# Attention's k-v product by head: two 65-column products on 64-column weight tiles in place of one 130-column product for a pair of heads

## What is computed

```python
q_s = exp(q - max(q, axis=-1)); q_s = q_s / (sum(q_s, axis=-1) + 1e-9)
k_s = exp(k - max(k, axis=2));  k_s = k_s / (sum(k_s, axis=2) + 1e-9)
kv  = np.einsum('bhsd,bhse->bhde', k_s, v)        # per head: 64x576 times 576x64
out = np.einsum('bhsd,bhde->bhse', q_s, kv)
# x = out as [4608, 512]
h = x @ w_in;  x = (h - tanh(h)) @ w_out           # [512, 2048], [2048, 512]
# then every row goes to the expert with the largest cosine, relu(x @ w1[e]) @ w2[e], times its gate
```

## Time and profile before

| | |
|---|---|
| median of 3 runs | 1547.14 us (1544.88 to 1548.52) |
| span of the profiled execution | 1546.1 us |
| TensorE matmul busy | 1464.8 us, 95% |
| TensorE weight load busy | 1275.8 us, 83% |
| VectorE busy | 979.8 us, 63% |
| ScalarE busy | 638.6 us, 41% |
| GpSimd busy | 406.7 us, 26% |

### The profile page before, as it was taken

One profiled execution on the slowest core, in us unless ns is written; L12 is line 12 of the kernel. 1 busy time (PEld: TensorE's weight loads), 2 busy tenths in 40 slices (PEclk: granted clock), 3 DMA queues, 4 the chain that ended last, 5 costly groups with the idle time before them and its releaser, 6 DMA issues.

```text
span 1546.1 us, 26526 instructions
## 1 busy us (share of the span) xinstructions
PE 1464.8 (95%) x7596; PEld 1275.8 (83%) x7597; DVE 979.8 (63%) x2003; ACT 638.6 (41%) x1268; POOL 406.7 (26%) x348
## 2 busy tenths in 40 slices
PE   4789999999999999999999999996999999999996
PEld 3678988989898988998898989985888888888885
DVE  8988677888778887867787876766422422432221
ACT  4454444455444454445444544443322322332220
POOL 3343233433323343323343332221000000001000
PEclk9799999999999999999999999997999999999999
DMA  8532011222001122101122000105421411411110
GB/s 194 145 93 78 1 45 31 57 49 54 16 15 48 33 64 47 45 2 45 31 55 51 23 14 14 62 15 183 148 78 43 142 48 41 146 41 41 47 39 25
DMA packets 139488, 90.85 MB, mean 59 GB/s; under 512 B 118872, under 2 KB 119128, under 8 KB 139232
## 3 DMA queue, kind: packets, MB, share of 16 engines
q1 hardware_dynamic: 132784, 70.12, 17.0%
q0 software_dynamic: 5840, 18.92, 3.2%
q10 hardware_dynamic: 736, 0.29, 0.1%
HBM read 70.39 MB, written 21.28 MB: 59 GB/s over the span
## 4 chain that ended last, share of the span: by engine, by line
PE 69%; DVE 19%; issue 6%; ACT 3%; POOL 0%; SPq 0%; DVEq 0%; DMA 0%; ACTq 0%; POOLq 0%
PE ps L510 20%; PE ps L511 20%; PE ps L512 20%; DVE gs L926 3%; DVE gs L923 2%; PE ps L683 2%; DVE big L921 2%; DVE gs L931 2%; PE ps L603 2%; PE ps L580 2%; DVE kfold L952 2%; DVE k_sb L960 1%; PE ps L597 1%; PE ps L662 1%; DVE qrec L945 1%
## 5 line engine op out<-in xcount | busy, mean ns | idle before, releaser
L1285 POOL TENSOR_TENSOR g_lo<-gs,g_hi 128x384 fp32r<-128x384 f32 x192 | 215.4, 1122 | 324.9 <-ACT g_hi L752 324.4
L510 PE MATMUL ps<-x_hi,wi_hi 128*128 128x384 f32 x768 | 279.8, 364 | 0.2 <-issue 0.2
L511 PE MATMUL ps<-x_lo,wi_hi 128*128 128x384 f32 x768 | 264.1, 344 | 0.0
L512 PE MATMUL ps<-x_hi,wi_lo 128*128 128x384 f32 x768 | 263.6, 343 | 0.0
L510 PE MATMUL ps<-wo_hi,g_hi 128*128 128x512 f32 x576 | 231.0, 401 | 13.4 <-POOL g_lo L1285 13.1
L511 PE MATMUL ps<-wo_lo,g_hi 128*128 128x512 f32 x576 | 229.4, 398 | 0.0
L512 PE MATMUL ps<-wo_hi,g_lo 128*128 128x512 f32 x576 | 227.8, 396 | 0.0
L752 ACT CAST g_hi<-gs 128x384 fp32r<-128x384 f32 x192 | 98.1, 511 | 287.2 <-DVE gs L931 285.3
L921 DVE TENSOR_SCALAR big<-usq 128x384 uint8<-128x384 f32 x192 | 117.0, 609 | 138.4 <-ACT usq L757 135.7
L861 ACT ACTIVATE hb<-ps 128x512 f32<-128x512 f32 x74 | 44.2, 597 | 314.6 <-PE ps L512 314.6
L1354 POOL DMA_INDIRECT out<-osb,xrow x37 | 36.2, 980 | 438.4 <-DVE osb L1258 429.5
(11 more groups left out here) (200 smaller groups left out, 2738.5 us busy)
## 6 DMA issues: line engine op xcount, KB each, us to landing
w_raw<-w SPq DMA_DIRECT2D x10, 2048.0 KB, 9.1
xrow<-scratch SPq DMA_DIRECT2D x37, 257.0 KB, 2.7
q_sb<-q SPq DMA_DIRECT2D x62, 144.0 KB, 2.9
k_sb<-k SPq DMA_DIRECT2D x62, 144.0 KB, 3.2
v_sb<-v SPq DMA_DIRECT2D x60, 144.0 KB, 3.3
in_raw<-w_in SPq DMA_DIRECT2D x8, 512.0 KB, 5.4
out_raw<-w_out SPq DMA_DIRECT2D x8, 512.0 KB, 5.4
scratch<-pad_d SPq DMA_DIRECT2D x8, 257.0 KB, 4.2
```

The lines of the kernel that those rows point to most:

```text
L510: mm(out_, a_hi, b_hi, start=first, stop=False)
L511: mm(out_, a_hi, b_lo, start=False, stop=False)
L512: return mm(out_, a_lo, b_hi, start=False, stop=last)
L1285: G.tensor_tensor(g_lo[:, (s - 1) % 3], gs[:, (s - 1) % 2], g_hi[:, (s - 1) % 3].bitcast(F32), ALU.subtract).then_inc(glo_ready, 1)
```

## The change

The weights of each step are the 64 columns of one head. The first head's product goes to partitions 0 to 63 of `bankA`, the second's to partitions 64 to 127, both into columns 0 to 64. v gets its ones per head: 64 columns and a one, twice (`HW` = 65, `VW` is still 130). There are 12 calls of `mm` in place of 6 for a unit. DVE reads the sums from column 64, and both blocks from columns 0 to 63. SP writes v of the second head one column further on. The ones are set by four instructions in place of two.

```diff
-VW = 2 * HD + 2
+HW = HD + 1
+VW = 2 * HW
@@ SP: load
-        def load(x_sb, x_d, x_in, u, par):
+        def load(x_sb, x_d, x_in, u, par, step=HD):
             x_in = arrived(x_in, u, par)[0]
             for h in range(2):
-                sp.dma_start(x_sb[:, :, h * HD:(h + 1) * HD],
+                sp.dma_start(x_sb[:, :, h * step:h * step + HD],
                              x_d[ds(u * 2 + h, 1)].rearrange("o (p r) d -> p (o r) d", r=R)).then_inc(x_in, 16)
@@ both calls for v
-            load(v_sb[:, par], v_d, v_in, u, par)
+            load(v_sb[:, par], v_d, v_in, u, par, HW)
@@ TensorE: kv
                 for r in range(R):
-                    last = mm(bankA[:, 0:VW], k_[:, r], v_[:, r, :], start=r == 0, stop=r == R - 1)
+                    for h in range(2):
+                        last = mm(bankA[h * HD:(h + 1) * HD, 0:HW], k_[:, r, h * HD:(h + 1) * HD],
+                                  v_[:, r, h * HW:(h + 1) * HW], start=r == 0, stop=r == R - 1)
                 last.then_inc(kv_ready, 1)
@@ DVE: kv
-                V.tensor_scalar_add(krec_[:, 0:1], bankA[:, 2 * HD:2 * HD + 1], 1e-9).then_inc(kv_step, 1)
+                V.tensor_scalar_add(krec_[:, 0:1], bankA[:, HD:HD + 1], 1e-9).then_inc(kv_step, 1)
...
-                    last = V.tensor_scalar(kv_[a, a], bankA[a, a], krec_[a, 1:2], None, ALU.mult)
+                    last = V.tensor_scalar(kv_[a, a], bankA[a, 0:HD], krec_[a, 1:2], None, ALU.mult)
@@ DVE: start
-        V.memset(qkv2[1][:, :, :, 2 * HD:VW], 1.0)
+        for h in range(2):
+            V.memset(qkv2[1][:, :, :, (h + 1) * HW - 1:(h + 1) * HW], 1.0)
...
-        V.memset(v_sb[:, :, :, 2 * HD:VW], 1.0).then_inc(zeroed, 1)
+        V.memset(v_sb[:, :, :, HW - 1:HW], 1.0)
+        V.memset(v_sb[:, :, :, VW - 1:VW], 1.0).then_inc(zeroed, 1)
```

More of the change, by code:

```diff
@@ L407, in _ @@
         for u in range(UPB):
-            load(unit_bufs(u, u % 2)[2], v_d, v_in, u, u % 2)
+            load(unit_bufs(u, u % 2)[2], v_d, v_in, u, u % 2, HW)
         load_piece(0)
```

## The result

Twenty executions of the changed kernel have a median of 1544.0 us (1541.1 to 1546.0), twenty of the kernel before 1548.6 (1543.5 to 1555.9). The ratio of the changed kernel to the kernel before is 0.9972, 95% interval 0.9962 to 0.9982: 4.3 us faster, between 2.8 and 5.9. The profiled span went from 1546.1 to 1541.7 us. The sum had said 9.4.

The account below looks back on a forecast made before the run. TensorE was taken to bound the walk (664.9 of 680 us). Units falling from 1.35 to 0.70 + 0.30 = 1.00 us, 27 times, save 9.4: 1546.1 - 9.4 + 1.0 = 1537.7, say 1538 us; range 1530 to 1561.

Parts of the forecast that it names:

- The sum: Product at line 580: a unit goes from 1.35 to 1.00 us; over 27 units of the walk, 9.4 us less.
- Streams and loads: Product at line 580: 56 ns per matmul and per 64-column load, two halves side by side, 0.70 us a unit.
- Switches: TensorE around the product: going to half-width and back costs 0.15 us each, 0.30 us a unit.
- Bare loads: Rival at line 580: loads can't run beside matmuls, 112 ns a pair, +44 us, 1591 us; chance 0.10.
- in turn: Rival at line 580: the halves alternate without overlap, 1.34 us a unit plus 0.30 for switches; chance 0.28.
- one after the other: Rival at line 580: streams of the two halves don't overlap, +8.1 us, 1555 us; chance 0.28.
- The rest costs nothing: DVE's kv work, extra settings of ones and v's transfers: no added time; the ones, if uncovered, 0.16 us.
- All 27 count: TensorE in the walk: each of 27 units' 0.35 us saving shows in full, 9.4 us; the other five count nothing.
- another engine turns out to hold the walk: Sign that the prediction is wrong: another engine bounds the walk once TensorE gets faster; no size given.
- The clock: Half-clock units after waits for the exponential: one or two more or fewer, 1.3 to 2.6 us either way.

Follow-up runs that it names:

- experiment 1: Changed kernel with the product's two loops exchanged, all six steps of one head, then the other's: 1553.0 us, ratio 1.0035 to the kernel before.
- experiment 2: Changed layout of v and its ones, but the full-width product of the kernel before: 1547.9 us, ratio 1.0003 to the kernel before.
- experiment 3: Changed kernel with POOL's scaling of q one slot later: 1537.4 us, ratio 0.9945 to the kernel before.
- filled kernel: Eight unread matmuls set into TensorE's 2.2 us waits for the exponential: kernel before 1542.2 us, changed kernel 1538.9.
- (7): Changed kernel with POOL's scaling one slot later and eight unread matmuls in the waits for the exponential: 1530.9 us, ratio 0.9902 to the kernel before.
- (8, 9): Kernel before with three of six row steps of the product, without and with POOL's scaling one slot later: 1560.0 us (1.0085) and 1551.9 (1.0033).
- edited kernels: POOL's scaling of q one slot later, in the changed kernel and in the kernel before: 1537.4 and 1545.9 us.

## Where the prediction held and where it failed

The forecast was 1538 us, 9.4 below the kernel before; 4.3 were measured. The direction, the two halves at work together and the size of the work saved held; that the walk turns this work into time one for one did not.

- *Streams and loads:* right. Two matmuls at a time, 58 ns a pair where 56 had been taken; 64-column loads last 132 to 138 ns, as the slope of the earlier trace rows had said (0.13 us). The rule of the Trainium skill, "TensorEngine Tiling (Array Packing)", section "Key Properties", that tiles load and multiply independently, agrees with the pairs and with experiment 1.
- *Switches:* right in size. The unit came to 1.00 to 1.05 us where 1.00 had been forecast; 0.09 us of that at the way in, as at line 635, the rest at the first pair and the way out. That section's rule of a drain agrees with these extra times, though no run isolates it.
- *Bare loads and in turn:* did not occur; the 24 loads of a unit ran beside its matmuls in 0.78 us. Experiment 1 gave the rival "one after the other" its measured price, +5.4 us where +8.1 had been worked out.
- *The rest costs nothing:* right (experiment 2).
- *"All 27 count":* this step failed. It took TensorE's 664.9 us of 680 and DVE's 542.3 to mean that no other engine is near enough. Busy shares of engines don't answer that. What counts is a chain, from DVE's sums over POOL's 1.49 us to `g_lo`, and in the kernel before it already held TensorE's reader, by 0.08 us at 299.19. In 12 of the 18 units of the table nothing of the shorter product arrived. POOL, the least busy engine (26%), held it, because it stood idle in its queue in front of an instruction whose input came late. The forecast had named the case "another engine turns out to hold the walk" as what would make it wrong, but gave it no price. What the runs show in place of "all 27 count": 9.4 us of work saved and 5.9 us of new waits in the profile, 4.4 of them for `g_lo`. Moving the scaling gave 4.2 to 6.6 us back, some 3.3 of it by the clock (experiment 3), and 8.0 us in the filled kernel, 1.4 by the clock (7). Half of the product showed new waits for `g_lo` as well (8, 9).
- *The clock:* taken as 1.3 to 2.6 us either way. The two profiles differ by 2.3 us there, and the filled kernels, with the same mean loss to the clock, lie 3.4 us apart where the unfilled ones lie 4.3 apart. That size held for this pair; between the edited kernels it was 4.5 us.

The version with the scaling one slot later beats both kernels at 1537.4 us. That this is close to the forecast of 1538 is in part luck, by the clock's share above. With the unread matmuls as well it is at 1530.9, 15.1 us or 1.0% under the kernel before.

## What to carry to other kernels

A saving on the bounding engine is worth what the next wait leaves of it: before it is counted in full, look at who delivers the reader's operands in each kind of slot, and by how little ahead of the reader. An in-order engine with a low busy share can be the bound if it stands in front of an instruction whose input comes late, with urgent work behind it; move that instruction behind the urgent one. Two products of 64 output rows each, issued in alternation, run side by side on the two halves of the array; in turn they don't.

## What the runs showed of the hardware

- Two float32 matmuls of 65 columns on different halves start 6 to 12 ns apart (nearly all pairs), and a pair takes 58 ns; on the same half each takes 57 to 60 ns. Their 64-column loads keep up: 24 of them ran beside 24 matmuls in 0.78 us.
- The way into half-width tiles cost 0.09 us, and a unit with both switches 0.30 to 0.35 us more than its streams.
- In the kernel before, each of the six waits of 2.2 us on TensorE between 220 and 900 us was followed by a stretch at half clock. It isn't so always: in the changed kernel with later scaling four of six waits of 2.3 to 2.4 us were. Eight unread matmuls in each such wait took the granted clock there from 0.98 to 1.00, and the time down by 3.7 us in the kernel before.
